# A gated-delta attention and two expert layers on one core: the first chunk's inversion, the order inside a block of 64, the router's steps and the last router rows

## The chip, the cores and the metric

The kernel runs on one core of a Trainium2 chip. A core has five engines with queues of their own: TensorE (PE, matmuls), VectorE (DVE), ScalarE (ACT), GpSimd (POOL) and SyncE (SP, which only issues DMAs here). The metric is the device time in microseconds of one execution. Before the change it is 1521.72 us, the median of 3 runs (1521.31 to 1523.83).

## The reference

```python
def _attn_ref(q, k, v, beta):            # q, k, v: (4, 8, 768, 48)
    k_n = k / (norm(k, axis=-1) + 1e-06)
    for t in range(S):
        y[:, :, t] = q_t @ state
        v_old = state^T @ k_n_t
        state = state + beta_t * outer(k_n_t, v_t - v_old)
def _moe_ref(x, domain_probs, w1, w2):   # x: (3072, 384), 4 experts of 1024
    out += p[:, e] * (relu(x @ w1[e]) @ w2[e])      # all experts, all tokens
def _moe2_ref(x, expert_emb, tau, w1, w2):          # 8 experts of 1024
    logits = xn @ en.T / tau ; expert_idx = argmax ; gate_w = softmax at the argmax
    out[mask] = gate_w[mask] * (relu(x[mask] @ w1[e]) @ w2[e])
```

## The kernel before, in words

**Attention in chunks.** The 768 steps of the recurrence are cut into 6 chunks of 128 tokens, and each chunk into two blocks (`ch`) of 64. With 32 heads that are 16 pairs, a chunk has 32 units of one pair and one block (`NU`). Inside a unit the recurrence is solved with matrices: the Gram matrix of keys times `gamma` gives `L` (`gram` on TensorE, `system` on VectorE), and the inverse of 1 + L is needed transposed, `TT`. The inverse is built from blocks of 32 (`BLK`). `diagonal` moves the four 32-row groups of the diagonal blocks into `Lblk` by transposes, `invert` on GpSimd runs 31 elimination steps of two operations each (62), every one waiting for the one before, and `back_transposed` and `back` transpose the results into `TT` and `Dn`. `first_products` and `second_products` form the off-diagonal block, `scores` and `masked` the masked products of keys and queries, `PT`. Then comes the scan over `UN` = 8 pieces of 4 pairs: `recalled`, `residual`, `solved`, `deltas`, `outputs` (of y and of the change of the state), `x_high`, `x_low` (y split into a high and a low half of reduced precision, `xhl`) and `state`. `move_x` copies 16-row pieces of `xhl` by 12 DMAs between partitions, so that a tile's x stands in three groups of 128 rows.

**Soft experts in steps.** A tile is 512 tokens, the four batches of one chunk, so tile t needs chunk t. It has 4 experts x 8 pieces of 128 hidden units, so 32 steps (`SPT`), and there are 6 tiles. Step n has `up(n)` (9 matmuls of 512 columns), then pieces of attention and of the router, then `down(n - 1)` (9 more). ScalarE makes the high half of each weight (`w_high`) two steps ahead, GpSimd the low half (`low`), and in steps in which GpSimd inverts, VectorE does (`w_low`; `inverting(m)` says which). `h_high` on ScalarE and `h_low` on VectorE read the hidden units. After each expert VectorE drains three banks (`drain`), and GpSimd adds the products of experts 1 and 2 (`add`, at steps 16 and 24 of the tile); VectorE adds those of the last.

**What sets the order.** Each engine runs one list of calls, written out over steps, and waits on semaphores. The attention for chunk t + 1 is done during tile t at step s = a + `LATE[t]`, so `LATE` shifts it within its tile, and GpSimd begins chunk t + 2's inversion at a = `INV_SLOT` = 20. The router works on the tile before: `route_rows` (four slices, one each at steps 1 to 4, transposes and logits), squares on ScalarE, `choices` at 7, `ranks` at 8, `places` at 9. The last tile's router stands after the last step, and after it the top experts: each tile of 256 tokens is gathered by an indirect DMA and goes through one expert.

**The start.** Chunk 0 is not beside any tile: its load, inversion (GpSimd) and scan come before `up(0)`, with Gram of chunk 1 between the pieces of the scan.

## Time and profile before

| what | value |
|---|---|
| median of 3 runs | 1521.72 us |
| the profiled execution, its own time | 1521.04 us |
| its span in the trace | 1519.3 us |
| first matmul of the soft experts | 132.84 us |
| last `hh` of the soft experts | 1171.35 us |
| first matmul of the top experts | 1218.09 us |
| TensorE busy | 1338.9 us (88%) |
| VectorE, ScalarE, GpSimd busy | 710.3, 457.5, 657.4 us |

Times in the trace run from the span's start. A name such as L1013 is line 1013 of the kernel. In a timeline row the number in front is the start, the next one the duration, and the text in brackets is how long the engine stood idle before and what released it. Matmuls overlap one another, so their distance says more than their duration. A busy share is an average over stages: what a stage costs is read from what TensorE waits for there.

### The profile page before, as it was taken

Reading aid. Unit: us, or ns where it says so; the run is one execution under the profiler, and the core shown is the slowest. Engines: PE = TensorE matmul, PEld = TensorE weight load, DVE = VectorE, ACT = ScalarE, POOL = GpSimd, SP = SyncE. Lnnn points to the kernel's source line nnn. Section 1 sums busy time; section 2 is a strip of 40 time slices with the busy share of each in tenths; the row PEclk is TensorE's granted clock in tenths of the full one; section 3 lists DMA queues with packets and bytes.
Section 4 is the critical chain, followed back from the end, with each engine's and each line's share of the span. In section 5 each row is a group of like instructions: output and inputs, shape, how many; then the busy total and the mean of one; then the engine's idle time right before and its main releaser. Section 6 shows DMA issues by size and latency. Waiting matters only on the chain. (4 is left out here: it accounts for less than half of the span.)

```text
span 1519.3 us, 30748 instructions
## 1 busy us (share of the span) xinstructions
PE 1338.9 (88%) x12639; PEld 1161.1 (76%) x12640; DVE 710.3 (47%) x1050; ACT 457.5 (30%) x790; POOL 657.4 (43%) x718
## 2 busy tenths in 40 slices
PE   1086999999999999969999799999999299999996
PEld 1085788877887778757888687888777299999996
DVE  5254644546536555535546445322452144444442
ACT  1012332233323333223322233333442133333231
POOL 4706442683328633492436823453554112223221
PEclk8578999999999999988999899999999589999998
DMA  8006222362234532352323232235333132343310
GB/s 181 26 3 141 80 80 71 119 153 73 76 97 131 129 70 64 112 142 81 63 92 101 80 91 71 70 118 191 102 102 131 31 115 89 128 142 129 128 38 22
DMA packets 66012, 146.69 MB, mean 97 GB/s; under 512 B 11252, under 2 KB 27057, under 8 KB 65320
## 3 DMA queue, kind: packets, MB, share of 16 engines
q1 hardware_dynamic: 53992, 114.69, 27.4%
q10 hardware_dynamic: 6912, 18.88, 3.7%
q0 software_dynamic: 4992, 11.44, 2.5%
q8 instruction: 89, 1.46, 0.4%
q14 instruction: 27, 0.22, 0.1%
HBM read 132.71 MB, written 11.48 MB: 95 GB/s over the span
## 5 line engine op out<-in xcount | busy, mean ns | idle before, releaser
L379 POOL TENSOR_TENSOR wsl<-raw,wsh 128x768 fp32r<-128x768 f32 x141 | 258.6, 1835 | 457.5 <-ACT wsh L475 457.1
L682 DVE SCALAR_TENSOR_TENSOR hl<-bank,hh 128x512 fp32r<-128x512 f32 x192 | 132.7, 691 | 473.5 <-ACT hh L479 469.7
L479 ACT ACTIVATE hh<-bank 128x512 fp32r<-128x512 f32 x192 | 114.8, 598 | 633.8 <-PE bank L1015 631.0
L1013 PE MATMUL bank<-xhl,wsh 128*128 128x512 f32 x576 | 227.1, 394 | 18.8 <-DMA xhl<-xhl 10.1
L1026 PE MATMUL bank<-hh,wsh 128*128 128x512 f32 x576 | 238.9, 415 | 4.2 <-DVE tmp L712 4.0
L1027 PE MATMUL bank<-hh,wsl 128*128 128x512 f32 x576 | 228.7, 397 | 0.0
L1028 PE MATMUL bank<-hl,wsh 128*128 128x512 f32 x576 | 228.0, 396 | 0.0
L1014 PE MATMUL bank<-xhl,wsh 128*128 128x512 f32 x576 | 226.3, 393 | 0.0
L1015 PE MATMUL bank<-xhl,wsl 128*128 128x512 f32 x576 | 226.1, 392 | 0.0
L475 ACT ACTIVATE wsh<-raw 128x768 fp32r<-128x768 f32 x192 | 160.7, 838 | 3.9 <-DMA raw<-in_w_soft 3.9
L1013 PEld LDWEIGHTS bank<-xhl,wsh 128*128 128x128 f32 x576 | 109.6, 190 | 43.2 <-issue 10.2
L370 POOL TENSOR_TENSOR outer<-Lblk,Tblk 128x31 f32<-128x31 f32 (+15 forms) x186 | 108.6, 584 | 75.9 <-DVE Lblk L617 61.8
L1026 PEld LDWEIGHTS bank<-hh,wsh 128*128 128x128 f32 x576 | 110.1, 191 | 29.6 <-issue 5.4
L1028 PEld LDWEIGHTS bank<-hl,wsh 128*128 128x128 f32 x576 | 110.4, 192 | 24.2
L1015 PEld LDWEIGHTS bank<-xhl,wsl 128*128 128x128 f32 x576 | 109.4, 190 | 23.0
L1014 PEld LDWEIGHTS bank<-xhl,wsh 128*128 128x128 f32 x576 | 109.4, 190 | 22.8
L1027 PEld LDWEIGHTS bank<-hh,wsl 128*128 128x128 f32 x576 | 110.4, 192 | 19.7
L373 POOL TENSOR_TENSOR Tblk<-Tblk,outer 128x31 f32<-128x31 f32 (+15 forms) x186 | 114.0, 613 | 14.6
L1293 PE MATMUL bank<-gh,wh 128*128 x384 | 110.3, 287 | 3.9 <-DVE gl L1236 2.4
L1295 PE MATMUL bank<-gh,wl 128*128 x384 | 109.9, 286 | 0.0
L1294 PE MATMUL bank<-gl,wh 128*128 x384 | 109.8, 286 | 0.0
L1242 DVE SCALAR_TENSOR_TENSOR hl<-bank,hh 128x512 fp32r<-128x512 f32 x64 | 44.2, 691 | 136.7 <-ACT hh L1205 108.3
(175 smaller groups left out, 2178.6 us busy)
## 6 DMA issues: line engine op xcount, KB each, us to landing
raw<-in_w_soft SPq DMA_DIRECT2D x192, 384.0 KB
rawT<-in_w_top ACTq DMA_DIRECT2D x48, 384.0 KB, 3.8
kq<-in_kq SPq DMA_DIRECT2D x12, 768.0 KB, 14.8
pb<-p_scratch SPq DMA_DIRECT2D x24, 256.0 KB, 3.7
rawT<-in_w_top SPq DMA_DIRECT2D x16, 384.0 KB, 7.3
kN<-in_kn SPq DMA_DIRECT2D x6, 768.0 KB, 5.8
vN<-in_vn SPq DMA_DIRECT2D x6, 768.0 KB, 4.8
xs_scratch<-xrow SPq DMA_DIRECT2D x24, 192.0 KB, 3.5
```

What stands on the lines that cost most here:

```text
L373: nc.gpsimd.tensor_tensor(T[:, m:BLK, 0:m], T[:, m:BLK, 0:m], o, ALU.subtract).then_inc(inv_step, 1)
L379: nc.gpsimd.tensor_tensor(wsl[:, n % WB, :], raw[:, n % RB, :], f32(wsh[:, n % WB, :]), ALU.subtract).then_inc(wlp_ok, 1)
L475: nc.scalar.activation(wsh[:, n % WB, :], raw[:, n % RB, :], ACT.Copy).then_inc(wh_ok, 1)
L479: nc.scalar.activation(hh[:, n % 2, :], ps_h[n % 2][:, :], ACT.Relu).then_inc(hi_ok, 1)
L682: nc.vector.scalar_tensor_tensor(out=hl[:, n % 2, :], in0=ps_h[n % 2][:, :], scalar=0.0, in1=f32(hh[:, n % 2, :]), op0=ALU.max, op1=ALU.su ...
L1013: nc.tensor.matmul(o, wsh[:, w, cols], x_hi, start=(kk == 0), stop=False)
L1014: nc.tensor.matmul(o, wsh[:, w, cols], x_lo, start=False, stop=False)
L1015: last = nc.tensor.matmul(o, wsl[:, w, cols], x_hi, start=False, stop=(kk == KM - 1))
L1026: nc.tensor.matmul(o, wsh[:, w, cols], hh[:, n % 2, :], start=(f == 0), stop=False)
L1027: nc.tensor.matmul(o, wsl[:, w, cols], hh[:, n % 2, :], start=False, stop=False)
L1028: last = nc.tensor.matmul(o, wsh[:, w, cols], hl[:, n % 2, :], start=False, stop=(f == NF - 1))
L1293: nc.tensor.matmul(o, wh[par][:, f, rows], x_hi, start=(kk == 0), stop=False)
```

## The change

Four things are changed.

**The start of chunk 0.** The DMAs come in another order: the embeddings first, then the keys alone (`load_features(0, 0)`), `kn`, v, and the queries after them. `invert(0)` runs on VectorE instead of GpSimd (the same function, given an engine). The scores and the Gram matrix of chunk 1 are computed ahead of it into other banks; ScalarE copies the scores, GpSimd masks them in one operation. The scan has two wide steps (one for each block of 64, in halves of 8 pairs) in place of 8 pieces; the first one leaves out the products with the state, which is zero. `move_x(0)` is split into halves. `invert(1)` stays on GpSimd, after the first two weight lows.

**The later half first.** Of each block of 64 tokens the later 32 are stored in the lower partitions. The two diagonal blocks of `L` then stand in the same columns, and one transpose of all 128 partitions does what four (or two) of 32 did. ScalarE copies the early block within `TT` (`move_early`, two a chunk). `gram` has a matmul of 64 and one of 32 columns for each head in place of one of 64.

**The table of steps.** `LATE` is [3, 1, 0, 0, 0, 0] in place of [7, 5, 3, 1, 0, 0], `INV_SLOT` 18 in place of 20, most attention calls stand one step earlier, and the router begins at step 3 (`ROUTE`).

**The last rows.** The four router slices of the last tile go to four banks. ScalarE only squares them, VectorE copies them out, and ScalarE loads its table for the square root ahead.

```diff
-    LATE = [7, 5, 3, 1, 0, 0]
-    INV_SLOT = 20
+    LATE = [3, 1, 0, 0, 0, 0]
+    INV_SLOT = 18
+    ROUTE = 3
...
-        return m < 9 or any(b <= m < b + 10 for b in begun)
+        return m < 6 or any(b <= m < b + 10 for b in begun)
...
+    def invert(eng, ops, c):
+        T = Tblk
+        flat = T[:, :, :].rearrange("p i j -> p (i j)")
+        first = INV_STEPS * c
+        if c:
+            eng.wait_ge(tb, 2 * c)
+        ops.memset(flat, 0.0).then_inc(inv_step, 1)
+        eng.wait_ge(inv_step, first + 1)
+        ops.memset(flat[:, 0:BLK * BLK:BLK + 1], 1.0).then_inc(inv_step, 1)
+        eng.wait_ge(inv_step, first + 2)
+        eng.wait_ge(tin, c + 1)
+        for s in range(BLK - 1):
+            n, m = BLK - 1 - s, s + 1
+            o = outer[:, 0:n * m].rearrange("p (n m) -> p n m", m=m)
+            ops.tensor_tensor(o, Lblk[:, s, m:BLK].unsqueeze(2).to_broadcast([P, n, m]),
+                              T[:, s:s + 1, 0:m].to_broadcast([P, n, m]), ALU.mult).then_inc(inv_step, 1)
+            eng.wait_ge(inv_step, first + 3 + 2 * s)
+            ops.tensor_tensor(T[:, m:BLK, 0:m], T[:, m:BLK, 0:m], o, ALU.subtract).then_inc(inv_step, 1)
+            if s < BLK - 2:
+                eng.wait_ge(inv_step, first + 4 + 2 * s)
...
+        sp.dma_start(en[:, :], emb).then_inc(e_in, 16)
+        sp.dma_start(taub[:, 0:1], tau.partition_broadcast(P)).then_inc(e_in, 16)
+        load_features(0, 0)
         load_kn(0)
         sp.dma_start(beta[:, :, :], beta_d).then_inc(b_in, 16)
-        load_kq(0)
         load_v(0)
-        sp.dma_start(pr[:, :, :], probs_d).then_inc(p_in, 16)
-        sp.dma_start(en[:, :], emb).then_inc(e_in, 16)
-        sp.dma_start(taub[:, 0:1], tau.partition_broadcast(P)).then_inc(e_in, 16)
+        load_features(0, 1)
+        load_features(1, 0)
         load_kn(1)
-        load_kq(1)
         for n in range(RB):
             load_raw(n)
-        sp.wait_ge(p_set, 1)
-        sp.dma_start(p_d, pr[:, :, :]).then_inc(p_out, 16)
+        sp.dma_start(pr[:, :, :], probs_d).then_inc(p_in, 16)
+        load_features(1, 1)
...
+        for half in range(NCH):
+            move_x(0, half)
...
+        mask_scores()
         for n in range(2):
-            if not low_by_vector(n):
-                low(n)
+            low(n)
+        invert(pool, nc.gpsimd, 1)
+        values(1)
...
+        def move_early(c, hh2):
+            if hh2 == 0:
+                act.wait_ge(tb, 2 * c + 1)
+                act.wait_ge(zero_set, ZEROS)
+            rows = ROWS_EARLY[hh2]
+            nc.scalar.activation(TT[rows, :, BLK:HALF], TT[rows, :, 0:BLK], ACT.Copy).then_inc(copied, 1)
...
+        def last_squares(j):
+            m = SUB * (NT - 1) + j
+            act.wait_ge(r_lg, m + 1)
+            if j == 0:
+                act.wait_ge(r_slot, NT - 1)
+                act.wait_ge(warm_ok, 1)
+            act.wait_ge(r_sx, m)
+            nc.scalar.activation(sqx[:, :], ps_last[j], ACT.Square, accum_out=sx[:, j:j + 1]).then_inc(r_sx, 1)
...
+        def diagonal(c):
+            dve.wait_ge(l_ok, VN * (c + 1))
+            if c:
+                dve.wait_ge(inv_step, INV_STEPS * c)
+            nc.vector.transpose(Lblk[:, :, :], L[:, :, 0:BLK].rearrange("p u s -> p s u")).then_inc(tin, 1)
...
+            nc.vector.transpose(TT[:, :, 0:BLK].rearrange("p u i -> p i u"), Tblk[:, :, :]).then_inc(tb, 1)
             if c:
                 dve.wait_ge(yy_mm, NCH * c)
-            for g in (0, 2):
-                rows = slice(BLK * g, BLK * g + BLK)
-                last = nc.vector.transpose(Dn[rows, :, :].rearrange("p u j -> p j u"),
-                                           Tblk[rows, :, :].rearrange("p i j -> p j i"))
-            last.then_inc(tb, 1)
+            nc.vector.transpose(Dn[:, :, :].rearrange("p u j -> p j u"),
+                                Tblk[:, :, :].rearrange("p i j -> p j i")).then_inc(tb, 1)
...
+        diagonal(0)
+        invert(dve, nc.vector, 0)
+        back(0)
         sums(1)
         norms(1)
+        for v in range(VN):
+            system(1, v)
+        diagonal(1)
+        for i in range(2):
+            wide_first_state(i)
+        for i in range(2):
+            wide_residual(i)
+        for ch in range(NCH):
+            for i in range(2):
+                wide_x_low(ch, i)
+        for i in range(2):
+            wide_state(i)
...
-                    k = kq[ROWS_D[hh2], c % 2, a0 + a, ch, 0, :]
-                    last = nc.tensor.matmul(dst[ROWS_T[hh2], a, :], k, k, start=True, stop=True)
+                    k = kq[ROWS_D[hh2], c % 2, 0, a0 + a, ch, :]
+                    nc.tensor.matmul(dst[ROWS_LATE[hh2], a, :], k[:, 0:BLK], k, start=True, stop=True)
+                for hh2 in range(2):
+                    k = kq[ROWS_D[hh2], c % 2, 0, a0 + a, ch, BLK:HALF]
+                    last = nc.tensor.matmul(dst[ROWS_EARLY[hh2], a, 0:BLK], k, k, start=True, stop=True)
...
+        for v in range(VN):
+            scores(0, v)
+        for v in range(VN):
+            gram(1, v)
         pe.wait_ge(mask_set, MASKS)
         pe.wait_ge(r_en, 2)
+        pe.wait_ge(pc_ok, VN)
         for kk in range(KM):
             last = nc.tensor.transpose(ps_en[:, E2 * kk:E2 * kk + E2], en2[:, kk * P:kk * P + P],
                                        identR[0:E2, 0:E2])
         last.then_inc(r_ent, 1)
-        pe.wait_ge(zero_set, ZEROS)
         first_products(0)
         second_products(0)
-        for v in range(VN):
-            scores(0, v)
-        for k in range(UN + 2):
-            if 1 <= k <= UN:
-                solved(0, k - 1)
-            if k < UN:
-                recalled(0, k)
-            if k >= 2:
-                outputs(0, k - 2)
-            if k in (2, 4):
-                gram(1, k - 2)
-                gram(1, k - 1)
-        pe.wait_ge(l_ok, 2 * VN)
-        pe.wait_ge(r_entc, 1)
+        for i in range(2):
+            wide_solved(0, i)
+        for i in range(2):
+            wide_changes(0, i)
+        for i in range(2):
+            wide_outputs(0, i)
+        for i in range(2):
+            wide_recalled(i)
+        for i in range(2):
+            wide_solved(1, i)
+        for i in range(2):
+            wide_outputs(1, i)
+        for i in range(2):
+            wide_changes(1, i)
...
-                if 1 <= s <= SUB:
-                    route_rows(t - 1, s - 1)
-                if s == 8:
+                if ROUTE <= s < ROUTE + SUB:
+                    route_rows(t - 1, s - ROUTE)
+                if s == ROUTE + 7:
                     ranks(t - 1)
```

On VectorE, at the start, from gamma of chunk 0 on, before (`Lblk` holds the diagonal blocks; L578 to L586 belong to the norms of chunk 1):

```order
L598 TENSOR_TENSOR gamma<-brn,norm 128x32
L607 TENSOR_TENSOR L<-bank,gamma 128x512 x4
L617 STREAM_TRANSPOSE Lblk<-L 32x1024 x4
L578 TENSOR_REDUCE ssq<-sq 128x32
L580 TENSOR_SCALAR ssq<-ssq 128x32
L584 RECIPROCAL rroot<-root 128x32
```

and after the change:

```order
L679 TENSOR_TENSOR gamma<-brn,norm 128x32
L688 TENSOR_TENSOR L<-bank,gamma 128x512 x4
L696 STREAM_TRANSPOSE Lblk<-L 128x1024
L239 MEMSET Tblk 128x1024
L241 MEMSET Tblk 128x32
L247 TENSOR_TENSOR outer<-Lblk,Tblk 128x31
L250 TENSOR_TENSOR Tblk<-Tblk,outer 128x31
L247 TENSOR_TENSOR outer<-Lblk,Tblk 128x60
```


The transposes are one, and the 62 operations of the inversion (three are shown) stand here; the norms of chunk 1 come behind them.

On VectorE, in the scan of chunk 0, before (`gks` and `R` are the residual, `xhl` the low half of y, `S` the state):

```order
L656 TENSOR_TENSOR gks<-bank,gamma 128x192
L661 TENSOR_TENSOR R<-vN,gks 128x192
L656 TENSOR_TENSOR gks<-bank,gamma 128x192
L661 TENSOR_TENSOR R<-vN,gks 128x192
L667 TENSOR_TENSOR xhl<-bank,xhl 112x4x64
L677 TENSOR_TENSOR S<-S,bank 112x192
L607 TENSOR_TENSOR L<-bank,gamma 128x512 x2
L656 TENSOR_TENSOR gks<-bank,gamma 128x192
L661 TENSOR_TENSOR R<-vN,gks 128x192
```


and after (`acc` holds the wide residual):

```order
L688 TENSOR_TENSOR L<-bank,gamma 128x512 x4
L696 STREAM_TRANSPOSE Lblk<-L 128x1024
L712 COPY S<-bank 112x384 x2
L723 TENSOR_TENSOR acc<-bank,gamma 128x384
L728 TENSOR_TENSOR acc<-vN,acc 128x384
L723 TENSOR_TENSOR acc<-bank,gamma 128x384
L728 TENSOR_TENSOR acc<-vN,acc 128x384
L733 TENSOR_TENSOR xhl<-bank,xhl 112x2x4x64 x4
L717 TENSOR_TENSOR S<-S,bank 112x384 x2
L817 TENSOR_REDUCE tmp<-tmp 24x128
```


The Gram of chunk 1 (L607 before, L688 after) is no longer between the pieces, and there is one round for each half of the pairs.

On GpSimd, from the lows behind the inversion of chunk 2 to the start of the inversion of chunk 3 in tile 1, before (L379 is the low weight half, L387 the addition of an expert, L353 v of the chunk, L393 the router's scatter):

```order
L379 TENSOR_TENSOR wsl<-raw,wsh 128x768 x6
L393 DMA slot_table<-payload,slot_i 24576x2 x4
L379 TENSOR_TENSOR wsl<-raw,wsh 128x768 x6
L387 TENSOR_TENSOR acc<-acc,tmp 128x512 x3
L379 TENSOR_TENSOR wsl<-raw,wsh 128x768 x8
L387 TENSOR_TENSOR acc<-acc,tmp 128x512 x3
L353 TENSOR_TENSOR vN<-vN,brn 128x1536
L362 MEMSET Tblk 128x1024
L364 MEMSET Tblk 128x32
L370 TENSOR_TENSOR outer<-Lblk,Tblk 128x31
```


and after (the same are L426, L434, L416 and L440), and, in a fence of its own, the end of that inversion with what follows it:

```order
L426 TENSOR_TENSOR wsl<-raw,wsh 128x768 x14
L440 DMA slot_table<-payload,slot_i 24576x2 x4
L426 TENSOR_TENSOR wsl<-raw,wsh 128x768 x4
L434 TENSOR_TENSOR acc<-acc,tmp 128x512 x3
L426 TENSOR_TENSOR wsl<-raw,wsh 128x768 x2
L416 TENSOR_TENSOR vN<-vN,brn 128x1536
L239 MEMSET Tblk 128x1024
L241 MEMSET Tblk 128x32
L247 TENSOR_TENSOR outer<-Lblk,Tblk 128x31
```


```order
L250 TENSOR_TENSOR Tblk<-Tblk,outer 128x2x30
L247 TENSOR_TENSOR outer<-Lblk,Tblk 128x31
L250 TENSOR_TENSOR Tblk<-Tblk,outer 128x31
L434 TENSOR_TENSOR acc<-acc,tmp 128x512 x3
L426 TENSOR_TENSOR wsl<-raw,wsh 128x768 x16
L440 DMA slot_table<-payload,slot_i 24576x2 x4
```


Before, both additions of a tile stand ahead of the inversion. After the change the second one stands behind it.

## Rows read from the trace of the kernel before

**Rows 1.** The page's part 2: granted clock in tenths, 40 slices of 38 us.
```profile
PEclk8578999999999999988999899999999589999998
```

**Rows 2.** Waits of TensorE, 132 to 1215 us: total, times, longest.
```profile
PE bank L1043 <- DVE acc L716: 24.7, 5, 14.6
...
PE bank L1013 <- POOL wsl L379: 8.0, 1, 8.0
...
PE bank L923 <- DVE TT L628: 4.4, 4, 2.3
...
PE bank L1026 <- DVE tmp L712: 4.0, 3, 2.0
```

**Rows 3.** Timeline, the start: start us, duration us, engine, line, operation, [idle before].
```profile
17.14 6.46 PE L907 MATMUL bank<-kq 48*64 48x64 f32 x128 [17.14 <-DMA kq<-in_kq]
...
24.36 7.59 DVE L617 STREAM_TRANSPOSE Lblk<-L 32x1024 f32<-32x1024 f32 x4
...
32.10 0.24 POOL L370 TENSOR_TENSOR outer<-Lblk,Tblk 128x31 f32<-128x31 f32 x1 [8.94 <-DVE Lblk L617]
...
69.31 0.25 POOL L373 TENSOR_TENSOR Tblk<-Tblk,outer 128x31 f32<-128x31 f32 x1
...
82.41 6.27 PE L947 MATMUL bank<-kq 48*64 48x64 f32 x128 [1.28 <-ACT TT L449]
...
123.61 7.58 SPq L256 DMA_DIRECT2D xhl<-xhl  x12
```

**Rows 4.** Timeline: one operation by size, GpSimd and VectorE.
```profile
19.30 2.76 POOL L353 TENSOR_TENSOR vN<-vN,brn 128x1536 f32<-128x1536 f32 x1 [11.38 <-DMA vN<-in_vn]
...
90.73 0.36 DVE L661 TENSOR_TENSOR R<-vN,gks 128x192 f32<-128x192 f32 x1
...
813.77 0.95 DVE L687 TENSOR_TENSOR wsl<-raw,wsh 128x768 fp32r<-128x768 f32 x1
```

**Rows 5.** Timeline of ScalarE: `hh` of successive steps, tiles 1 and 4.
```profile
307.62 0.60 ACT L479 ACTIVATE hh<-bank 128x512 fp32r<-128x512 f32 x1 [2.75 <-PE bank L1015]
...
311.70 0.60 ACT L479 ACTIVATE hh<-bank 128x512 fp32r<-128x512 f32 x1 [2.75 <-PE bank L1015]
...
321.97 0.60 ACT L479 ACTIVATE hh<-bank 128x512 fp32r<-128x512 f32 x1 [4.88 <-PE bank L1015]
...
327.10 0.60 ACT L479 ACTIVATE hh<-bank 128x512 fp32r<-128x512 f32 x1 [2.95 <-PE bank L1015]
...
856.77 0.60 ACT L479 ACTIVATE hh<-bank 128x512 fp32r<-128x512 f32 x1 [2.75 <-PE bank L1015]
...
878.59 0.60 ACT L479 ACTIVATE hh<-bank 128x512 fp32r<-128x512 f32 x1 [4.89 <-PE bank L1015]
```

**Rows 6.** Timeline: the inversion that starts in tile 3.
```profile
811.88 0.60 ACT L479 ACTIVATE hh<-bank 128x512 fp32r<-128x512 f32 x1 [2.75 <-PE bank L1015]
...
814.75 4.05 DVE L617 STREAM_TRANSPOSE Lblk<-L 32x1024 f32<-32x1024 f32 x2
...
818.95 0.24 POOL L370 TENSOR_TENSOR outer<-Lblk,Tblk 128x31 f32<-128x31 f32 x1 [4.05 <-DVE Lblk L617]
...
861.04 0.25 POOL L373 TENSOR_TENSOR Tblk<-Tblk,outer 128x31 f32<-128x31 f32 x1
...
861.25 3.70 POOL L387 TENSOR_TENSOR acc<-acc,tmp 128x512 f32<-128x512 f32 x3
```

**Rows 7.** Timeline of TensorE: half a chunk of Gram, and first products.
```profile
270.39 2.08 PE L907 MATMUL bank<-kq 48*64 48x64 f32 x64
...
346.83 2.21 PE L923 MATMUL bank<-TT,L 32*32 32x32 f32 x128 [1.36 <-DVE TT L628]
```

**Rows 8.** Timeline: router slices of the last tile.
```profile
1180.14 0.90 PE L1043 MATMUL bank<-identR,acc 128*128 128x128 f32 x3 [1.05 <-ACT sqx L495]
...
1183.17 0.90 PE L1043 MATMUL bank<-identR,acc 128*128 128x128 f32 x3 [1.05 <-ACT sqx L495]
...
1189.21 1.28 ACT L499 ACT_TABLE_LOAD   x1
```

More of the change, by code:

```diff
@@ L55, in program @@
     LIVE = slice(0, HALF + D)
+    ROWS_LATE, ROWS_EARLY = (tuple(slice(HALF * hh2 + BLK * q, HALF * hh2 + BLK * q + BLK) for hh2 in range(2))
+                             for q in range(2))
     def sb(stack, name, shape, dt=F32):
@@ L931, in second_products @@
                 for a in range(NPAIR):
-                    for hh2 in range(2):
-                        top = slice(HALF * hh2, HALF * hh2 + BLK)
-                        last = nc.tensor.matmul(ps_z[ch][top, a, :], Dn[top, NPAIR * ch + a, :],
-                                                z1[top, NPAIR * ch + a, :], start=True, stop=True)
+                    for rows in ROWS_EARLY:
+                        last = nc.tensor.matmul(ps_z[ch][rows, a, :], Dn[rows, NPAIR * ch + a, :],
+                                                z1[rows, NPAIR * ch + a, :], start=True, stop=True)
                 last.then_inc(yy_mm, 1)
@@ L948, in scores, with wide_solved @@
             last.then_inc(p_mm, 1)
+        def wide_solved(ch, i):
+            if ch == 0:
+                pe.wait_ge(copied, 2)
+                pe.wait_ge(yy_ok, NCH)
+                pe.wait_ge(v_ok, 1)
+            else:
+                pe.wait_ge(r_ok, NB * (i + 1))
+                pe.wait_ge(u_ok, 2 * i + 2)
+            for a in range(8):
+                for rows in ROWS_T:
+                    u = NPAIR * ch + 8 * i + a
+                    rhs = wide_R[rows, 8 * i + a, :] if ch else vN[rows, u, :]
+                    last = nc.tensor.matmul(wide_u[i][rows, a, :], TT[rows, u, :], rhs, start=True, stop=True)
+            last.then_inc(u_mm, 2)
@@ new lines, in wide_changes @@
+        def wide_changes(ch, i):
+            pe.wait_ge(u_ok, NB * ch + 2 * i + 2)
+            if ch == 0:
+                pe.wait_ge(l_ok, VN + i + 1)
+            else:
+                pe.wait_ge(s_ok, 2 * i + 2)
+            for a in range(8):
+                for hh2 in range(2):
+                    last = nc.tensor.matmul(wide_ds[i][ROWS_D[hh2], a, :], kN[ROWS_T[hh2], 0, NPAIR * ch + 8 * i + a, :],
+                                            wide_U[ROWS_T[hh2], ch, 8 * i + a, :], start=True, stop=True)
+            last.then_inc(wide_ds_mm, 1)
```

430 lines of the change are left out of this document (244 added, 186 removed).

## The prediction

> **What bounds the kernel now.** I read the clock line and the busy slices first: outside the two dips at the start and near slice 31, TensorE is busy nine tenths or more at the full clock [rows 1], so a change pays only where TensorE stands still, or where it gets less or more to do. The waits of TensorE over the main loop and the step after it name the places [rows 2]: 24.7 us for the sum of expert outputs that the router reads (`acc`), 8.0 us for low weight halves from GpSimd, 4.0 us for drained banks, 4.4 us for transposed inverses. I then read the timeline of the start: the first matmul of the soft experts comes at 132.84 us, and what precedes it is one chain [rows 3]: keys landed at 17.1, Gram scaled, four quarter transposes of 7.59 us together, GpSimd's inversion from 32.1 to 69.6 (37.5 us), products until 82.4, scores and the scan until 123.6, twelve copies of x of 7.58 us with their landing. Last come the intervals between starts of `hh` on ScalarE, one for each step of 1/32 tile: a bare step is 4.08 us (307.62 to 311.70), one with a router slice 5.13 (321.97 to 327.10) [rows 5].
>
> **The start, term by term.** Keys come first and alone now, 0.79 MB in place of 1.57, with `kn` behind them; as 2.45 MB took until 17.1 us [rows 3], I put `kn` at about 13, the squares, norms and gamma at 18, and L at 21.5. One transpose of 128 rows replaces four of 32. Rows 3 price a quarter at 1.9 us. The lanes work side by side in other operations, so I take one quarter's time, and four quarters (7.6) as the other end. With Tblk's memsets the inversion starts at 25.
>
> Its 62 operations move to VectorE. The trace has 0.36 us for 192 elements a lane and 0.95 for 768 [rows 4]; the line through both is 0.16 + n/970 us. The 62 have 2 x 5456 elements: 62 x 0.16 + 11.2 = 21.1 us, and some 0.035 us between dependent ones makes 23.3, against GpSimd's 37.5. Beside it GpSimd masks the scores and takes two weight lows, by its own rate (2.76 us for 1536 elements [rows 4]) 3.7 + 3.7 = 7.4 us. Those share operands' memory with VectorE's. In the inversion of tile 3, GpSimd's chain took 42.3 us in place of 37.5 while VectorE did ten lows of about 0.95 [rows 3, 6]: half of the other engine's time was added. So contention costs 3.7 to 7.4 here, and I take 7.4, since here GpSimd's operations are the long ones and a short one of VectorE waits for a whole one. The inversion ends at 55.5.
> The Trainium skill says more in "SBUF — State Buffer", section "Who interferes with whom": the pair of ports is an exclusive lock, and the loser is blocked for the whole instruction. By that rule the term is 7.4, by the ratio of rows 3 and 6 it is 3.7, and the sum would be 3.7 us lower by the latter.
>
> Then 2.0 for the transpose into TT and, as before from TT to the start of scores (73.5 to 82.4 less half a microsecond of transposes), 8.4 more: 65.9. The scores, which took from there to 89.5, lie ahead of the inversion's end now, behind the q load. The scan in two wide steps has 96 matmuls of 64 columns and 160 of 48; at 98 ns each as in scores (64 in 6.27 us at the low clock [rows 3]) and three quarters of that for 48 columns, TensorE has 21 us at the low clock and 11 at the high; hand-overs between the engines, about ten of 0.6 us, come on top. I take 23 (17 to 29): x is complete at 89. The copies of the second half then take what they took, 9.3 us from the last low of x to the first matmul [rows 3]; those of the first half issue during the scan. First matmul at 98, **35 us earlier** (28 to 43). The next inversion, on GpSimd, runs from 69 to about 110 and is asked for at step 4 of tile 0, near 118, so it is hidden; if it were not, each microsecond would count once. In tile 0 the first products waited 2.3 us for it and fell to the low clock; that step took 11.8 us against 6.3 elsewhere: **5.5 us** go.
>
> **The main loop.** The router's slices move from steps 1 to 4 to steps 3 to 6. The wait for `acc` goes with it: in tile 1, step 1 took 10.27 us in place of 5.13 [rows 5], 5.1 lost, of which 3.3 is the wait and 1.8 the low clock behind it. The same in tile 2 (5.0), 1.3 in tile 5. In tile 3 it is 14.6 us of wait and 4.0 of clock, since the inversion that began at step 23 held the addition of step 24 on GpSimd until 679. In tile 4 the lows were late by 8.0 us and two steps lost 12.6 in all (856.77 to 878.59 is 21.8, against 4.08 + 5.13 [rows 5]). Sum of what the old schedule loses there: 5.1 + 5.0 + 18.6 + 12.6 + 1.3 = **42.6 us**.
>
> This is where I expect most to come back. The inversions of chunks 2 to 5 start at steps 27, 25, 23 and 21 of their tiles now, and at 21, 19, 18, 18 after the change. GpSimd is in order, so every one of the four then has the addition of step 24 behind it, and behind that the low for step b + 12, where b is the step at which it starts; VectorE makes only the ten lows b + 2 to b + 11. All steps from b to b + 12 are bare steps of 4.08. That is what tile 3 did before with b = 21. There `hh` of step b began at 811.9, the second pair of quarter transposes ended at 818.8, the chain ended at 861.3, the additions at 865.0, the low at 866.7 [rows 6], and TensorE, done at 858.7, waited 8.0 us [rows 2]. After the change one transpose stands in step b in place of two, and it starts sooner, which brings the chain 2.3 us forward: 5.7 us of wait remain. The clock behind it cost 1.8 us after a wait of 3.3 and 4.6 after one of 8.0; I take 3.0. Four tiles x 8.7 = **34.8 us come back** (none, if the chain were 5.7 us shorter; 4 x 12.6 = 50 if nothing is gained on tile 3 of before).
>
> Gram has four matmuls a pair in place of two: 64 columns and 32 columns for each head. The trace shows 2.08 us for half a chunk with 64 columns [rows 7], so 4.16 a chunk, and half more is 2.1 a chunk. All of it is on TensorE: **+8.3 us** for four chunks. For 32 columns the trace has 128 matmul rows in 2.21 us, 17 ns each, half of the 33 of 64 columns [rows 7], so columns set the price.
> The Trainium skill, "TensorE: Matmul & The Clock Gate", section "Wait — 56ns, not 53.3ns?", says that starts are never closer than about 25 ns however few the columns. The trace disagrees with that for these small tiles (17 ns). By that figure the term would be 512 x 25 ns = 12.8, and the sum 4.5 us higher.
>
> With a third of the transposes left in a chunk (3 in place of 10), the waits of first products for TT (1.4 + 0.4 + 0.4) and of TensorE for drained banks (4.0 in all [rows 2], VectorE being in transposes) go: **6.1 us**. ScalarE gets two copies of 1.1 us a chunk; it waits 2.75 us of each bare step of 4.08 [rows 5], so they cost nothing; without that cover, 2.2 us a chunk.
>
> **The tail.** The last tile's four router slices stood one after the other, each behind 1.05 us for the square of the slice before, at a pitch of 3.03 us [rows 8]. With four banks the pitch is TensorE's own 3.03 - 1.05 = 2.0, which saves 3 to 5 us; the table load of 1.28 [rows 8] is ahead of it, and VectorE's copy of the last rows adds 0.3. **5 us** (3 to 7) go.
>
> Sum against the profiled execution's own 1521.04: -35 - 5.5 - 42.6 + 34.8 + 8.3 - 6.1 - 5 = -51.1, or 1469.9. The median of the runs shown is 0.7 above that execution, so I say **1470**.
>
> **Rivals.**
> *No new waits.* If the inversion is done within twelve steps, the 34.8 stay away: 1435. For it: fewer transposes, and the end is missed by 5.7 us only, of which the 3.7 of additions could have come before. Against: the order on GpSimd puts the additions behind in all four tiles, and the 42.3 us of chain repeats in all of them. 0.14.
> *The inversion is no quicker on VectorE.* If dependent steps cost it 0.6 us, as they cost GpSimd (37.5 / 62), or the lock costs more, the start gains 15 to 20 in place of 35: 1488. For it: the operands are broadcast and strided, which no row of VectorE shows at this size; against: rows of 32 elements follow each other at 0.22 us. 0.14.
> *The wide transpose costs four quarters.* Then each inversion starts 5.8 us later: 4 x 7 in the tiles, and 17 at the start: 1515. For it: no row has more than 32 partitions; against: the operations of 128 partitions in rows 4 lie on one line of elements a lane. 0.05.
> *The other side: inversions pushed into every tile's end make it slower.* The late low for step b + 12 holds TensorE in four tiles in place of one; it costs more than all gains from 21.5 us a tile (8.7 + 51/4) on, that is with a wait of about 17 us, as in tile 3 of before, where the sum of wait and clock was 18.6. If each of the four lost 23, it would be 1527. For it: 14.6 us is on record [rows 2]. Against: that wait came from a start at step 23, with TensorE stopped by the addition; here the start is earlier and the router two steps later. 0.03.
> The forecast has 0.62, and 0.02 is for anything else.
>
> **How the numbers follow.** The forecast's own range is 1455 to 1485, from the start (7 either way), the four waits (0 to 15 more) and the clock. For 8 in 10 I add half of the two cases beside it: 1440 to 1492. A measurement of this kernel can tell about 0.2% from no change; faster by more than that holds everything but the fourth rival and a part of the wide transposes: 0.96; same 0.01; slower 0.03.
>
> **What would show it.** First soft matmul near 98 us; 62 operations of 0.34 us mean on VectorE before 56; no wait of the router's transposes for `acc`; four waits of 5 to 6 us of the first `up` matmul for GpSimd's `wsl`, in tiles 0 to 3 at step 33 (that is, 1 of the next), 31, 30 and 30, with a lower granted clock behind them; Gram at 6.2 us a chunk; 2.0 us a slice in the tail. It is wrong if the four waits are absent or above 10 us, or if the first soft matmul lies outside 88 to 105.

## The result and the profile after

The changed kernel takes **1469.56 us**, the median of 4 runs (1467.1 to 1472.87), against 1521.51 (1519.53 to 1523.83). The ratio is **0.9668**, with a 95% interval of 0.9647 to 0.9689: 3.3% faster. Predicted were 1470 and 1440 to 1492. The profiled execution took 1468.24 us, with a span of 1466.5.

| stretch | before, us | after, us | difference | predicted |
|---|---|---|---|---|
| to the first matmul of the soft experts | 132.84 | 97.90 | -34.9 | -35 |
| from there to the last tile's first router row | 1045.1 | 1032.9 | -12.2 | -11.1 |
| from there to the first transpose of the top experts | 36.2 | 31.5 | -4.7 | -5 |
| the top experts | 305.1 | 304.2 | -0.9 | 0 |

The four add up to -52.7. Each came out within 1.1 us of its term. The first two did so only because errors of both signs met in them, which the sections below take apart.

The clock line of the page's part 2, changed kernel, slices of 37 us, answers to [rows 1]:
```profile
PEclk7579999999999999989999999999999599999998
```
The clock line differs in a few digits only. At this scale the gain can't be seen; it has to be read from the waits.

Waits of TensorE from 98 to 1133 us in the changed kernel (total, times, longest), to be read against [rows 2]:
```profile
PE bank L1168 <- POOL wsl L426: 24.5, 5, 5.9
...
PE bank L1030 <- issue: 3.5, 2, 2.1
PE bank L1211 <- DVE oh L867: 3.3, 1, 3.3
PE bank L1168 <- DVE wsl L783: 3.1, 2, 2.9
PE bank L1203 <- DVE acc L812: 2.6, 1, 2.6
```
L1203 holds the router's transposes (L1043 before). Their wait for `acc` has gone from 24.7 us to the 2.6 of the last tile. The wait for low halves from GpSimd has gone from 8.0 to 24.5, nearly all of it four equal waits of 5.9. The waits for `TT` and `tmp` are gone or small. Two lines have no counterpart in the prediction: second products (L1030) that stop for "issue", which is time in which the engine waited for nothing that the profile shows, and the ranks of tile 5 (L1211).

Timeline of the start, changed kernel, answering to [rows 3]:
```profile
22.12 1.94 DVE L696 STREAM_TRANSPOSE Lblk<-L 128x1024 f32<-128x1024 f32 x1
25.35 0.19 DVE L247 TENSOR_TENSOR outer<-Lblk,Tblk 128x31 f32<-128x31 f32 x1
...
30.04 0.36 DVE L250 TENSOR_TENSOR Tblk<-Tblk,outer 128x192 f32<-128x192 f32 x1
30.12 4.66 POOL L421 TENSOR_TENSOR PT<-PT,upper 128x2048 f32<-128x2048 f32 x1 [10.72 <-ACT PT L509]
...
30.43 4.57 DVE L247 TENSOR_TENSOR outer<-Lblk,Tblk 128x207 f32<-128x207 f32 x1
...
34.74 3.83 POOL L426 TENSOR_TENSOR wsl<-raw,wsh 128x768 fp32r<-128x768 f32 x2
35.04 1.86 DVE L250 TENSOR_TENSOR Tblk<-Tblk,outer 128x207 f32<-128x207 f32 x1
36.94 1.88 DVE L247 TENSOR_TENSOR outer<-Lblk,Tblk 128x220 f32<-128x220 f32 x1
...
57.85 3.46 PE L1020 MATMUL bank<-TT,L 32*32 32x32 f32 x122 [17.33 <-DVE TT L704]
...
79.09 17.30 SPq L312 DMA_DIRECT2D xhl<-xhl  x24
...
97.90 0.77 PE L1168 MATMUL bank<-xhl,wsh 128*128 128x512 f32 x1 [12.19 <-DMA xhl<-xhl]
```
One transpose of 128 rows takes 1.94 us. The inversion runs from 25.35 to 55.9 us. Three of its operations show how the two engines meet: 207 elements take 4.57 us where 192 take 0.36. The operation began 0.3 us behind the start of GpSimd's masks and ended 0.2 us behind their end; the next two ended 0.2 us behind GpSimd's two lows. Together they lost 7.2 us. SyncE issues the 24 copies of x from 79.1 to 96.4 us, 1.5 us before the first soft matmul.

Timeline of the turn from tile 0 to tile 1, changed kernel, answering to [rows 6]; the `hh` rows are those of steps 0 and 1 of tile 1:
```profile
270.69 0.60 ACT L546 ACTIVATE hh<-bank 128x512 fp32r<-128x512 f32 x1 [2.75 <-PE bank L1170]
...
272.85 0.25 POOL L250 TENSOR_TENSOR Tblk<-Tblk,outer 128x31 f32<-128x31 f32 x1
273.06 3.70 POOL L434 TENSOR_TENSOR acc<-acc,tmp 128x512 f32<-128x512 f32 x3
...
276.72 3.59 POOL L426 TENSOR_TENSOR wsl<-raw,wsh 128x768 fp32r<-128x768 f32 x2
...
278.58 0.79 PE L1168 MATMUL bank<-xhl,wsh 128*128 128x512 f32 x1 [5.89 <-POOL wsl L426]
...
282.82 0.60 ACT L546 ACTIVATE hh<-bank 128x512 fp32r<-128x512 f32 x1 [10.80 <-PE bank L1170]
```
The same three in a row as in [rows 6], chain, additions, low, and TensorE stands behind the low. The granted clock is read from the windows view (length, busy time of each engine, then the clock, DMA share and GB/s):
```profile
272.70:278.50 5.80, 0.00 (x0) 0.00 (x0) 1.65 (x3) 0.00 (x0) 5.72 (x7) 0.81 0.00 1
278.50:282.60 4.10, 4.02 (x10) 3.15 (x11) 3.56 (x4) 0.00 (x0) 1.81 (x2) 0.50 0.76 262
```
After 5.8 us without a matmul the next 4.1 us run at the low level, 1.2 GHz. So the two steps take 12.1 + 4.3 us in place of 2 x 4.08: 8.2 us for a wait of 5.9. The other three are alike (448.63, 626.30 and 807.26 us), with 12.1 + 4.5 or 4.6.

Timeline of the last tile's router slices, changed kernel, answering to [rows 8]:
```profile
1130.80 0.55 PE L1203 MATMUL bank<-identR,acc 128*128 128x128 f32 x3 [2.58 <-DVE acc L812]
...
1131.77 0.52 PE L1203 MATMUL bank<-identR,acc 128*128 128x128 f32 x3
...
1134.29 0.88 PE L1203 MATMUL bank<-identR,acc 128*128 128x128 f32 x3
```
The first two pitches are 0.97 and 0.95 us, since nothing stands between the slices; the last is 1.57, when the granted clock has fallen. The fourth slice starts 3.5 us behind the first, where it took 8.2 before (1177.97 to 1186.21).

### The profile page after: what moved, and what is told of

Read it like the earlier page. It is cut to its first block and busy times, and to the rows that moved or that the text cites. A ratio compares the mean times of both kernels' runs of the same rounds, so it can differ in the third digit from the quotient of the medians.

```text
span 1466.5 us, 32008 instructions
## 1 busy us (share of the span) xinstructions
PE 1333.5 (91%) x13279; PEld 1156.4 (79%) x13280; DVE 640.5 (44%) x1048; ACT 470.8 (32%) x794; POOL 632.9 (43%) x660
## 5 line engine op out<-in xcount | busy, mean ns | idle before, releaser
L426 POOL TENSOR_TENSOR wsl<-raw,wsh 128x768 fp32r<-128x768 f32 x146 | 267.9, 1837 | 469.2 <-ACT wsh L542 468.9
L1168 PE MATMUL bank<-xhl,wsh 128*128 128x512 f32 x576 | 229.9, 399 | 39.8 <-POOL wsl L426 24.5
L1169 PE MATMUL bank<-xhl,wsh 128*128 128x512 f32 x576 | 228.3, 396 | 0.0
L542 ACT ACTIVATE wsh<-raw 128x768 fp32r<-128x768 f32 x192 | 160.7, 838 | 11.1 <-DMA raw<-in_w_soft 11.0
L250 POOL TENSOR_TENSOR Tblk<-Tblk,outer 128x31 f32<-128x31 f32 (+15 forms) x155 | 99.0, 639 | 12.1
L247 POOL TENSOR_TENSOR outer<-Lblk,Tblk 128x31 f32<-128x31 f32 (+15 forms) x155 | 86.7, 559 | 34.1 <-DVE Lblk L696 22.3
## 6 DMA issues: line engine op xcount, KB each, us to landing
kq<-in_kq SPq DMA_DIRECT2D x24, 384.0 KB, 11.3
```

Source lines behind the costliest of these rows:

```text
L426: nc.gpsimd.tensor_tensor(wsl[:, n % WB, :], raw[:, n % RB, :], f32(wsh[:, n % WB, :]), ALU.subtract).then_inc(wlp_ok, 1)
L542: nc.scalar.activation(wsh[:, n % WB, :], raw[:, n % RB, :], ACT.Copy).then_inc(wh_ok, 1)
L1168: nc.tensor.matmul(o, wsh[:, w, cols], x_hi, start=(kk == 0), stop=False)
L1169: nc.tensor.matmul(o, wsh[:, w, cols], x_lo, start=False, stop=False)
```

## The experiments

Edits are to the changed kernel unless said otherwise. The kernel before measured 1514.6 to 1517.8 us beside these runs, so each is judged by its ratio to it. A difference to the changed kernel is the difference of the two ratios times 1521.5 us. Each ratio is known to about 3 us, so differences under some 4.5 us are told by the traces alone.

### Do the four waits come from what is queued behind the inversion?

```diff
-        return m < 6 or any(b <= m < b + 10 for b in begun)
+        return m < 6 or any(b <= m < b + 13 for b in begun)
```
VectorE makes three more lows for each inversion (13 in place of 10).


> The changed kernel, with VectorE making 13 low weight halves beside an inversion in place of 10. Theory (each of the four inversions leaves the low for step b + 12 behind itself and the addition on GpSimd, and TensorE waits 5.9 us for it, with 2.6 us of low clock behind): the waits of the soft up matmuls for GpSimd go, 12.1 + 4.5 us of steps become 2 x 4.08, four times 8.4 us: 1469.6 - 33.6 = 1436. Rival (the waits only move, since VectorE then is late with hl or the lows): 1455 or more, with waits for VectorE in steps b + 12 to b + 15.


Measured: 1438.32 (1435.38 to 1441.13), ratio 0.9491 (0.9466 to 0.9515), 27 us less. Waits of TensorE, 98 to 1133 us, three more lows on VectorE:
```profile
PE bank L1181 <- DVE tmp L808: 4.9, 2, 4.1
PE bank L1030 <- issue: 4.2, 2, 2.2
...
PE bank L1168 <- POOL wsl L426: 1.0, 1, 1.0
```
The wait for GpSimd's lows fell from 24.5 to 1.0 us, and the four pairs of steps are bare ones of 4.1. What is missing to the 33.6 expected stands in the first two lines. GpSimd still adds the products of expert 2 behind the inversion, at 273.1; until it has read `tmp`, VectorE can't drain a bank into it, and the next `down` stood still for 4.1 us (step 1 of tile 1 took 10.8). The stops for "issue" stayed in their places, and those steps took 12.6 and 14.3 us (11.3 and 10.6 in the changed kernel). Together that is 11.7 us lost; 4.0 came back in tile 5, mostly because TensorE waited 1.6 us for the ranks in place of 3.35.

The same edit with `b + 11`, one more low:


> The changed kernel with 11 lows on VectorE in place of 10, a dose between. Theory: the first low on GpSimd is then due one step (4.08 us) later, so the wait is 5.9 - 4.1 = 1.8 us, too short for the clock to fall (2.0 us of standstill did not make it fall before, 3.3 did): 4 x (8.4 - 1.8) = 26 us less than the changed kernel, 1443. Rival as for thirteen: 1455 or more.


Measured: 1447.95 (1439.31 to 1450.75), ratio 0.9542 (0.9504 to 0.9579), 19 us less. Three waits are left, of 2.19, 2.45 and 1.99 us, where 1.8 was expected; at the fourth place TensorE waited 3.6 us for `tmp`. Timeline and windows at the first of them:
```profile
447.87 0.47 PE L1168 MATMUL bank<-xhl,wsh 128*128 128x512 f32 x1 [2.19 <-POOL wsl L426]
```
```profile
447.80:450.60 2.80, 2.73 (x9) 2.24 (x10) 0.00 (x0) 0.00 (x0) 1.61 (x1) 0.73 0.52 156
```
The expectation had the clock wrong: behind the waits of 2.19 and 1.99 us it did fall to the low level, about 1.2 and 0.8 us after TensorE had started again, and the two steps lost 4.1 and 3.9 us over bare ones. Behind the 2.45 it stayed at full speed, and 2.8 were lost, as it had stayed behind 2.04 us in the kernel before (459.93). The theory of the queue holds in both runs: each low taken off GpSimd's queue shortens the wait.

### What is the new table of steps worth?

```diff
-    LATE = [3, 1, 0, 0, 0, 0]
-    INV_SLOT = 18
+    LATE = [7, 5, 3, 1, 0, 0]
+    INV_SLOT = 20
```


> The changed kernel with the step table of before: LATE = [7, 5, 3, 1, 0, 0] and INV_SLOT = 20, so that inversions start at steps 27, 25, 23 and 21; the router stays at step 3. Theory (the new table costs, since all four starts lie before the addition of step 24): the first two waits go (2 x 8.4), the third becomes one for drained banks or the router's sum of 12 to 15 us with 3 to 4 of clock, the fourth stays: 33.6 - 25 = 8 us faster than the changed kernel, 1461. Rival (the new table is worth something beside that, by the transposes and the scan being spread better): 1475 or slower.


Measured: 1448.15 (1446.02 to 1452.3), ratio 0.9569 (0.9547 to 0.959), **15 us less** than with the new table. Timeline of TensorE, the old table in the new kernel:
```profile
623.73 0.76 PE L1181 MATMUL bank<-hh,wsh 128*128 128x512 f32 x1 [9.28 <-DVE tmp L808]
...
798.09 0.79 PE L1168 MATMUL bank<-xhl,wsh 128*128 128x512 f32 x1 [4.08 <-POOL wsl L426]
```
Three waits in place of four (the first of 3.13 us at 459.54), and no stops for "issue". In tiles 0 and 1 the inversion begins after step 24, so the addition is not behind it at all. The new table is the one part of the change that was found to lose. With 13 lows it does better than the old one with 10 (0.9491 against 0.9569); the old table with 13 lows was not run, so which table is the better one then is open. The old table also shows the other form of the same fault: begun at step 23, the inversion holds the addition, the addition holds `tmp`, and TensorE waits 9.28 us.

### Was it the router's shift that removed its waits?

The kernel before, with all router work of a tile two steps later and nothing else:
```diff
-                if 1 <= s <= SUB:
-                    route_rows(t - 1, s - 1)
-                if s == 8:
+                if 3 <= s < 3 + SUB:
+                    route_rows(t - 1, s - 3)
+                if s == 10:
```


> The kernel before with one part of the change alone: the router's calls two steps later (rows at steps 3 to 6, choices 9, ranks 10, places 11). Theory: the waits for the sum of experts in tiles 1, 2 and 5 go, with the low clock behind them (5.1 + 5.0 + 1.3), and of tile 3's 18.6 only 2 to 3, because TensorE then stands at the drained banks for the same addition: 13 us faster than before, 1508. Rival (the whole 42 us of these waits go by this part alone): 1480.


Measured: 1510.43 (1508.35 to 1516.76, 10 runs), ratio 0.9975 (0.9958 to 0.9993): 4 us, where 13 was expected. Timeline of TensorE, the kernel before with the router shifted:
```profile
506.66 0.50 PE L1013 MATMUL bank<-xhl,wsh 128*128 128x512 f32 x1 [4.33 <-POOL wsl L379]
...
674.86 0.77 PE L1026 MATMUL bank<-hh,wsh 128*128 128x512 f32 x1 [11.71 <-DVE tmp L712]
```
The waits for `acc` inside the loop were gone, and TensorE waited for other work of the same two engines: 2.4 us for a drained bank in tile 1, 4.3 us for a low in tile 2, 11.7 us for `tmp` in tile 3, where it had waited 14.6 for `acc` [rows 2].

The reverse in the changed kernel, the router back at steps 1 to 4:
```diff
-    ROUTE = 3
+    ROUTE = 1
```


> The changed kernel with the router back at step 1 of the tile (ROUTE = 1). Theory: TensorE waits for the sum of experts again where it did before, 5.1 us a tile with the clock in tiles 2, 3 and 4, nothing in tile 1 (it stands for the low there already), 1 to 4 in tile 5: 14 us slower than the changed kernel, 1484. Rival (with fewer transposes VectorE has the sum in time, so the shift of the router is worth nothing): 1470.


Measured: 1469.63 (1465.2 to 1471.16), ratio 0.9684 (0.9668 to 0.97), 2 us more, which is no difference: the time is the rival's. Waits of TensorE, 98 to 1133 us, `ROUTE` = 1:
```profile
PE bank L1203 <- DVE acc L812: 6.7, 5, 2.6
PE bank L1211 <- DVE oh L867: 5.4, 4, 1.8
```
The `acc` waits in tiles 2 to 5 are 1.03 us each, not 3.2 to 14.6. In the kernel before, GpSimd was inverting until step 5 of tile 1, 3 of tile 2 and 1 of tile 3, and in tiles 1 and 2 VectorE's three additions into `acc` took 2.95 and 2.99 us beside it; here, with no inversion there, 1.98. The kernel before has the control in itself: in its tile 5, with no inversion, they took 1.98 and TensorE waited 1.03. So the traces speak for it that the `acc` waits shrank because the inversion no longer runs across a tile's first steps; that fewer transposes had a part is not excluded. Nor was the shift worth nothing everywhere: `ROUTE` = 1 brought back the four waits of 1.03 and two of 1.8 us for ranks, and spared the stops for "issue" (2.10 and 1.43) and 1.75 us of the wait for ranks in tile 5.

### The start: who should invert, and what runs beside it?

GpSimd inverts chunk 0, ahead of the masks (`invert(0)` called on that engine instead of VectorE):
```diff
+        invert(pool, nc.gpsimd, 0)
...
-        invert(dve, nc.vector, 0)
```


> The changed kernel with chunk 0's inversion on GpSimd again, ahead of the masks and the two lows there. Theory: it takes 37.5 us as before against the 30.5 us that VectorE took, blocked 7.2 us by GpSimd's masks and lows; the masks and lows now come after it and hide behind the products: 7 us slower than the changed kernel, 1477. Rival (the move to VectorE is worth what its unblocked speed says, 37.5 - 23.3): 14 us slower, 1484.


Measured: 1472.93 (1469.41 to 1477.02), ratio 0.9698 (0.9668 to 0.9727), 4.6 us more. First products begin at 62.67 us instead of 57.85 and the first soft matmul comes at 102.68 instead of 97.90. So the choice of engine is worth 4.8 us. GpSimd's chain took 36.6 us here (from 24.07), undisturbed. VectorE's is 13.3 us quicker by itself (23.3, next run) and loses 7.2 of that to the masks and lows beside it; and it starts 1.3 us later (25.35), since VectorE has to clear `Tblk` behind the transpose, which GpSimd does ahead of it.

The masks and lows wait for the inversion instead:
```diff
+            pool.wait_ge(tb, 1)
```


> The changed kernel with GpSimd's masking of the scores and its two lows made to wait until VectorE's inversion of chunk 0 is transposed. Theory (GpSimd's operations held the memory port, and three of VectorE's 62 operations took 8.3 us in place of 1.1): the inversion takes 23.3 us, the first soft matmul comes 7.2 us earlier, the masks (3.7 us) are done before the first outputs: 1462.4. Rival (the three long operations have another cause, or the masks are then late for the scan): 1467 to 1473.


Measured: 1461.77 (1460.33 to 1464.88), ratio 0.9636 (0.9612 to 0.966), 4.9 us less. Timeline, masks behind the inversion:
```profile
43.51 0.38 DVE L247 TENSOR_TENSOR outer<-Lblk,Tblk 128x207 f32<-128x207 f32 x1
...
51.34 3.46 PE L1021 MATMUL bank<-TT,L 32*32 32x32 f32 x122 [9.60 <-DVE TT L705]
...
90.91 0.76 PE L1169 MATMUL bank<-xhl,wsh 128*128 128x512 f32 x1 [13.49 <-DMA xhl<-xhl]
```
The operations of 207 elements take 0.37 and 0.38 us now, the whole chain takes 23.3 in place of 30.5, and the first products and the first soft matmul come 6.5 and 7.0 us sooner. The three blocked operations, 7.2 us, were all of the loss, and the masks were in time when they began at 51.4. The Trainium skill has the rule in "SBUF — State Buffer", section "Who interferes with whom": the pair of ports that VectorE shares with GpSimd is an exclusive lock, and a VectorE instruction with two SBUF inputs contends with a GpSimd instruction that reads SBUF. The trace agrees, 4.57 us against 0.37, and shows the other side too. In the whole trace of the changed kernel, 57 `TENSOR_TENSOR` operations of VectorE with both inputs in SBUF (the memory that the engines share) began while one of GpSimd of over 0.9 us was under way, and not one ended before it. Of 104 that read one input from a bank of PSUM (the memory that TensorE writes) instead, none took over 0.02 us longer than the quickest of its kind.

`move_x(0)` whole, with 12 DMAs instead of 24:
```diff
-        for half in range(NCH):
-            move_x(0, half)
+        move_x(0)
```


> The changed kernel with the copies of chunk 0's x between partitions issued once for whole rows (12 DMAs after the last piece) in place of two halves (24 DMAs). Theory (SyncE's queue is the path: 24 issues of 0.72 us from 79.1 us on, while x is complete at 85.8): the first soft matmul comes at 85.8 + 9.3 = 95.1 in place of 97.9, 2.8 us faster, 1466.8. Rival (the landing of the last copies is the path, so halves help): 1470 to 1474.


Measured: 1467.4 (1456.88 to 1473.3), ratio 0.9682 (0.9653 to 0.9712), unclear by the time. By the trace the first soft matmul comes at 93.91 us behind a wait of 9.37, instead of 97.90 behind 12.19. The split costs 2.8 us of wait (the other 1.2 us came before it): at 0.72 us an issue (17.30 / 24), SyncE was not through the first half's copies when the second half was ready. In the other runs with the split this wait was 12.5 to 13.7 us, and in the one without it (the last run) 9.3, so the split costs 2.8 at the least.

### Is the added Gram work on TensorE's path?

The matmuls of the early half, 32 columns, are done twice for chunks 2 to 5:
```diff
-                for hh2 in range(2):
+                for hh2 in 2 * (0, 1) if c >= 2 else (0, 1):
```


> The changed kernel with the 32-column Gram matmuls of chunks 2 to 5 done twice (they overwrite the same result). Theory A, the prediction's price (each costs its columns, 17 ns a row of the trace): 4 x 2.1 = 8.3 us slower, 1478. Theory B (they run beside the 64-column ones in other columns of the array, as the unchanged step time of 6.2 us suggests): less than 2 us slower, 1470 to 1472.


Measured: 1474.78 (1473.28 to 1477.12), ratio 0.9714 (0.9694 to 0.9735), 7 us more. It looks like theory A, but the trace shows another thing. A chunk's two Gram steps took 6.2 + 6.2 us before the doubling; now they take 6.5 + 7.3, 6.5 + 8.1, 6.5 + 11.8 and 6.5 + 8.5. The doubled matmuls cost 0.3 us where nothing else happens; the rest is in the second steps alone. Timeline of TensorE, Gram twice, the second steps of chunks 2 and 4:
```profile
219.95 0.19 PE L1005 MATMUL bank<-kq 48*32 48x32 f32 x1 [0.62 <-issue]
...
572.03 0.27 PE L1005 MATMUL bank<-kq 48*32 48x32 f32 x2 [2.26 <-issue]
```
TensorE stopped amid small matmuls, for nothing that the profile shows. So neither theory is right: the work is nearly free, and stops of another kind come with dense small matmuls.

The DMA queues hold a trace of what they are. Queue q8, which the profile names `instruction`, brings in code. Timeline of TensorE, and the DMA view (packets, MB) of the window 472.3 to 472.5, changed kernel, at the stop of 2.10 us:
```profile
474.91 0.76 PE L1030 MATMUL bank<-z,Dn 32*32 32x32 f32 x37 [2.10 <-issue]
```
```profile
q8 instruction: 1, 0.02, 33.8%
```
That packet of 16 KB started at 472.39 and had landed at 473.48, and TensorE went on 1.43 us later. The same holds at all 20 stops of over 0.3 us in the second products and Gram of the main loop, in the eight traces of the changed kernel and its variants that have any: each ended 1.23 to 1.49 us behind the landing of such a packet, which only 3% of all moments do. So TensorE most likely had run out of instructions and waited for the next packet; small matmuls use them up fastest (one every 17 ns in [rows 7]). No run tests this. It doesn't cover the six shorter stops in the scores and the scan of the kernel before (0.3 to 1.8 us) nor the one of `ROUTE` = 1 (1.21), which came 4.8 us or more behind a packet.

### The three gains together

`b + 13`, the masks behind the inversion, and `move_x(0)` whole (the three diffs above).


> The changed kernel with three edits together: 13 lows on VectorE, the masks and first lows after the inversion of chunk 0, the copies of x for whole rows. If they add up (33.6 + 7.2 + 2.8): 1426. If the start's two gains overlap, 1428 to 1430.


Measured: **1429.8** (1427.51 to 1431.27), ratio 0.9422 (0.9406 to 0.9438): 37 us faster than the changed kernel and 5.8% faster than the kernel before. The first soft matmul comes at 86.46, behind a wait of 9.3 us for the copies. The 43.6 expected are short by the same two things as in the first experiment: TensorE waited 4.9 us for `tmp`, 4.1 of it in tile 1, and stopped for "issue" for 4.2 us.

## Why the prediction came out, point by point

**The start (-35, measured -34.9).** The transpose (1.9 predicted, 1.94), the inversion (25 to 55.5 predicted, 25.35 to 55.9) and its blocking (7.4 predicted, 7.2) were right, and the run with the masks behind the inversion shows the last of these directly. Then two errors cancelled. I had x complete at 89; it was at 85.8 (85.07 + 0.69), since the scan in wide steps was 3.2 us quicker. And I took 9.3 us for the copies behind it; they took 12.1, because I charged only the second half's twelve issues and forgot that SyncE was still issuing the first half's. That they cancelled is luck. And 2.7 us were there to be had: TensorE stopped for "issue" for 5.67 us within Gram of chunk 0 (up to 20.24, 1.39 behind a packet of instructions), and VectorE waited 2.70 us for its last bank.

**Tile 0 (-5.5, measured -2.0).** The step of 11.8 us is gone, as said. But TensorE waited 2.94 us for a low of VectorE (121.96), and three steps there took 17.3 us. VectorE was not the late one. Timeline, tile 0 of the changed kernel:
```profile
120.07 0.84 ACT L542 ACTIVATE wsh<-raw 128x768 fp32r<-128x768 f32 x1 [6.53 <-DMA raw<-in_w_soft]
...
121.96 0.50 PE L1168 MATMUL bank<-xhl,wsh 128*128 128x512 f32 x1 [2.94 <-DVE wsl L783]
```
ScalarE waited 6.53 us for a weight to land. SyncE had issued it at 104.46, 6.6 us behind the first soft matmul, which is no later than before (7.1); but it took 15.6 us to land, against 12.8 (139.90 to 152.71). Ahead of it in the queue now stand the first two loads of `pb` and v of chunk 1 as well, 1.3 MB, which SyncE issues at 98.2 and 99.3, behind the copies of x, and before the change issued ahead of them (41.0 and 117.8). No run moves them alone, so that they are the cause is argued. The number of copies is not: with 12 of them the wait was 3.39 us. I had no term for any of this.

**What the old schedule lost (-42.6, by the steps -41.3).** It is gone: the router's wait for `acc` and GpSimd's late low with it. The sum was 1.3 too high, since tile 3 lost 17.3 us (a step of 22.4, from 671.88 to 694.28, in place of 5.13) and not 18.6. Part of its reason was wrong. I said the `acc` waits go because the slices stand two steps later. The run with `ROUTE` = 1 and the shifted router in the old kernel show that the shift alone brings 4 us there and nothing here.

**The four waits (+34.8, measured +33.7).** Four waits of 5.9 us (5.7 predicted), two steps of 12.1 + 4.3 to 4.6 us each, 8.2 to 8.6 lost (8.7 predicted), at the four places named. This was the step on which most hung, and it came from reading one instance in the old trace and asking where its pattern would repeat.

**Gram (+8.3, measured -0.4).** This step failed. A Gram step takes 6.25 us, as it did before (6.32). Windows view of the main loop, first of the kernel before, then of the changed one:
```profile
133.00:1178.00 1045.00, 995.95 (x9294) 822.63 (x9294) 511.42 (x732) 339.37 (x587) 523.86 (x503) 0.98 0.36 102
```
```profile
98.00:1131.00 1033.00, 994.24 (x9807) 821.37 (x9808) 438.09 (x697) 353.59 (x599) 507.96 (x478) 0.98 0.38 104
```
TensorE has 513 more matmuls and is busy 1.7 us less. The lines view gives the shapes (changed kernel, 190 to 1135 us):
```profile
L1002 PE MATMUL bank<-kq 48*32 48x64 f32 x512 | 15.8, 217 | 0.0
L1005 PE MATMUL bank<-kq 48*32 48x32 f32 x512 | 14.7, 202 | 0.0
```
The weights are 48 x 32 now and were 48 x 64 [rows 7]. A matmul fills half as much of the array, and their rows in the timeline lie over one another: 15.8 + 14.7 us busy in eight steps that exceed bare ones by 17.4 us in all. I had counted columns streamed as if each matmul ran alone. That the smaller share of the array is what lets them run side by side fits this and the 0.3 us of the doubled ones, but no run varies the width alone.

**VectorE's waits (-6.1, by the steps -5.7).** The waits for `TT` went, and 2.6 of the 4.0 for `tmp`. No run takes the single transposes back alone, so their share in this is argued.

**Not foreseen.** Two stops for "issue" at the second products in tiles 2 and 3 (2.10 and 1.43 us, with the clock 3.9 and 3.2). But the kernel before had such stops too, in the scan and the scores, with 6.0 us of longer steps in all, and they went. Waits of TensorE, 132 to 1215 us, kernel before:
```profile
PE bank L997 <- issue: 1.8, 1, 1.8
PE bank L993 <- issue: 1.5, 4, 0.5
```
So the stops make a difference of 1.1 us only. And in tile 5 there is a wait of 3.35 us for the ranks, where there had been 1.62. Timeline of tile 5, changed kernel:
```profile
1027.35 1.82 DVE L651 TENSOR_TENSOR nx<-sx,nx 128x4 f32<-128x4 f32 x1
...
1031.40 1.80 POOL L426 TENSOR_TENSOR wsl<-raw,wsh 128x768 fp32r<-128x768 f32 x1 [2.24 <-ACT wsh L542]
1031.49 1.75 DVE L867 TENSOR_TENSOR oh<-key,mk 128x32 bf16<-128x32 f32 x1
1033.30 0.19 PE L1211 MATMUL bank<-oh,after 128*128 128x40 bf16 x1 [3.35 <-DVE oh L867]
```
Four elements a lane take 1.82 us. It is the blocking of the start again: a short operation of VectorE that began just behind a low of GpSimd waited for its end.

The main loop, read from the intervals between starts of `hh`:

| part | predicted | measured |
|---|---|---|
| tile 0 | -5.5 | -2.0 |
| losses of the old schedule | -42.6 | -41.3 |
| the four waits | +34.8 | +33.7 |
| Gram | +8.3 | -0.4 |
| waits for `TT` and `tmp` | -6.1 | -5.7 |
| stops for "issue" | 0 | +1.1 |
| ranks and one low in tiles 1 and 5, the state in tile 1 | 0 | +4.0 |
| all other steps of attention | 0 | -1.6 |
| sum | -11.1 | -12.2 |

Gram and the other steps of attention cost 10.3 us less than predicted, and the other rows together 9.2 more. The total is right to 0.5 us; the main loop is right by cancelling, which is luck.

**The tail (-5, measured -4.7).** As said, though by other sizes: the ranks came 6.1 us sooner behind the first slice (9.4 us in place of 15.5), and from there to the first gathered tile it took 1.4 us longer.

**The rivals.** *No new waits* was what the experiment with `b + 13` made of it, at 27 us and not 34.8. *Inversion no quicker* and *four quarters* are refuted by 0.36 us for 192 elements and 1.94 for the transpose. *Slower* needed waits of 17 us; they were 5.9.

## What to carry to other kernels

When a long chain goes onto an engine that works in order, list what stands behind it for the next dozen steps, and move those calls as well as the chain: here 13 instead of 10 lows elsewhere was worth 27 us, more than half of what the whole change gave. A saved wait counts only once the next one in the same buffers is known: a late addition showed as a wait for `acc`, for `tmp` or for a low, by where the router stood. For small matmuls look at the shape of the weights before pricing by columns.

## What the runs showed of the hardware

A `TENSOR_TENSOR` of VectorE with both inputs in SBUF that starts behind one of GpSimd of over 0.9 us waits for its end, however small it is: 4.57 us instead of 0.37, 1.82 us for four elements, and 57 of 57 cases in one trace. One that reads a bank of PSUM does not (104 of 104). A dependent chain of 62 such operations takes 23.3 us on VectorE free of this, and 36.6 to 37.5 on GpSimd. A transpose of 128 x 1024 takes 1.94 us, no more than one of 32 x 1024 (1.9). Matmuls with 32 columns of weights run nearly free beside others of their kind: 512 more cost nothing that shows. Behind waits of 1.99 and 2.19 us TensorE ran at the low clock for some time, as behind 5.9; behind 2.04 and 2.45 it did not. Its stops for "issue" amid dense small matmuls ended 1.2 to 1.5 us behind the landing of a 16 KB packet of instructions, 20 times of 20. In every run with the new table and the router at step 3 they came at the same two places, step 3 of tiles 2 and 3 (0.5 to 2.5 us); with `ROUTE` = 1 there was one of another kind elsewhere (1.21 us), with the old table none, and with Gram doubled four more. So the order of the instructions has a part in them; that TensorE waits for instructions is the likely cause, not a tested one.
